# Gram products of two chunks on four corners of the array instead of two

## What is computed

```python
k_n = k / (np.linalg.norm(k, axis=-1, keepdims=True) + 1e-06)
state = np.zeros((B, H, D, D))
for t in range(S):
    kt, vt, bt = (k_n[:, :, t], v[:, :, t], beta[:, :, t, None])
    y[:, :, t] = einsum('bhd,bhde->bhe', q[:, :, t], state)
    v_old = einsum('bhde,bhd->bhe', state, kt)
    state = state + bt[:, :, :, None] * einsum('bhd,bhe->bhde', kt, vt - v_old)
x = y as (B * S, H * D)
# experts: out[mask] = gate_w * eom * (relu(x[mask] @ w1[e]) @ w2[e]), e = argmax(x @ w_gate)
# last layer: maximum(x @ w1, x @ w2, x @ w3) @ w_out
```

## Time and profile before

| | us |
|---|---|
| median of three runs | 1061.64 |
| the runs | 1056.43 to 1076.32 |
| the profiled execution | 1061.8 |
| its span | 1060.1 |
| attention stage, without its start and end | 60 to 420 |
| TensorE busy over the span | 1008.5 (95%) |
| vector engine busy | 522.3 (49%) |
| ScalarE busy | 375.6 (35%) |
| GpSimd busy | 364.0 (34%) |

### The profile page before, as it was taken

One profiled execution on the slowest core, in us unless ns is written; L12 is line 12 of the kernel. 1 busy time (PEld: TensorE's weight loads), 2 busy tenths in 40 slices (PEclk: granted clock), 3 DMA queues, 4 the chain that ended last, 5 costly groups with the idle time before them and its releaser, 6 DMA issues. The chain is left out here.

```text
span 1060.1 us, 28043 instructions
## 1 busy us (share of the span) xinstructions
PE 1008.5 (95%) x11748; PEld 883.5 (83%) x11748; DVE 522.3 (49%) x1109; ACT 375.6 (35%) x735; POOL 364.0 (34%) x275
## 2 busy tenths in 40 slices
PE   3899999999999999789999999998999999999998
PEld 3788888888888888669999999997788888888987
DVE  5567667775677765354444443442433333323332
ACT  3556566565566666122222222221312121212110
POOL 4545376554535342133564552634301010100000
PEclk9899999998999999689999999999999999999999
DMA  9222222221222120234542445322201010100000
GB/s 302 100 57 60 58 75 66 67 67 50 65 68 67 51 60 17 95 130 172 179 171 92 149 154 171 134 90 82 60 30 34 26 37 22 37 30 8 23 8 30
DMA packets 58044, 84.66 MB, mean 80 GB/s; under 512 B 28880, under 2 KB 52944, under 8 KB 55376
## 3 DMA queue, kind: packets, MB, share of 16 engines
q1 hardware_dynamic: 52272, 46.89, 14.3%
q0 software_dynamic: 5664, 36.18, 9.9%
HBM read 61.62 MB, written 21.43 MB: 78 GB/s over the span
## 5 line engine op out<-in xcount | busy, mean ns | idle before, releaser
L1159 PE MATMUL hb<-early,last_h 128*128 128x512 f32 x648 | 206.0, 399 | 0.5 <-DVE early L1303 0.5
L1159 PEld LDWEIGHTS hb<-early,last_h 128*128 128x128 f32 x648 | 120.4, 189 | 28.3 <-DVE early L1303 0.9
L1159 PE MATMUL hb<-early,last_l 128*128 128x512 f32 x324 | 128.4, 396 | 0.0
L750 POOL TENSOR_TENSOR n_base<-n_kb_a,cf 128x512 f16<-128x512 f32 x24 | 30.4, 1268 | 167.8 <-DVE n_kb_a L600 167.8
L610 DVE TENSOR_TENSOR p<-bank,cf 128x512 f16<-128x512 f32 x96 | 66.2, 690 | 36.0 <-PE bank L379 34.9
L552 ACT CAST t<-bank 128x512 f16<-128x512 f32 x96 | 56.5, 588 | 66.4 <-PE bank L372 66.1
L1196 POOL DMA_INDIRECT rows<-y_sorted,idx x24 | 24.5, 1022 | 155.1 <-PE ob L1227 151.8
L1159 PE MATMUL ob<-wo_h,early 128*128 128x384 f32 x288 | 75.1, 339 | 0.0
L1083 POOL TENSOR_TENSOR late<-w_raw,late 128x3072 fp32r<-128x3072 f32 x8 | 54.5, 6811 | 59.8 <-DVE late L1023 59.5
L1159 PEld LDWEIGHTS hb<-early,last_l 128*128 128x128 f32 x324 | 61.0, 188 | 14.8
L992 ACT CAST ht_h<-ht_bank 128x512 fp32r<-128x512 f32 x56 | 32.9, 587 | 109.4 <-PE ht_bank L943 55.4
(11 more groups left out here) (173 smaller groups left out, 2205.4 us busy)
## 6 DMA issues: line engine op xcount, KB each, us to landing
w_raw<-w POOLq DMA_DIRECT2D x14, 1536.0 KB, 7.7
kq_t<-qh SPq DMA_DIRECT2D x24, 256.0 KB
y_sorted<-y_sb SPq DMA_DIRECT2D x31, 192.0 KB, 1.9
x_in<-x_sorted SPq DMA_DIRECT2D x29, 192.0 KB, 2.5
k_raw<-kt_in SPq DMA_DIRECT2D x24, 192.0 KB, 2.4
v_in<-vh SPq DMA_DIRECT2D x24, 192.0 KB
k_own<-kh SPq DMA_DIRECT2D x24, 192.0 KB, 2.4
out<-o_sb SPq DMA_DIRECT2D x24, 192.0 KB, 1.8
```

The lines of the kernel that those rows point to most:

```text
L1159: ins = pe.matmul(out, a[x], b[y], start=first and i == 0, stop=last and i == 2, skip_group_check=True)
```

## The change

In `gram` the loops over e and p are exchanged, and the second chunk's head half hh writes to the other partition half, `half[hh ^ e]`. The matmuls of a pair now go to the corners (0, 0), (1, 1), (0, 1) and (1, 0) in turn. Both signals are given in the last turn. For chunk 1 everything that follows has its two heads in swapped partition halves: the keys, values and beta on the host (`crossed`), beta_k, the views from which rhs is formed, and z. As the zeros of z lie in other places for chunk 1, z gets one buffer per chunk.

```diff
+    def crossed(x, heads, chunks):
+        second = np.flip(x, heads)
+        return np.where(np.arange(2).reshape([2 if i == chunks else 1 for i in range(x.ndim)]) == 1, second, x)
+
+    kh = crossed(k.transpose(g, s, st, hh, t, e, p, d), 3, 5).reshape(TILES, P, U, D)
+    vh = crossed(v.transpose(g, s, st, hh, t, e, p, d), 3, 5).reshape(TILES, P, 2, NP, D)
+    bh = np.stack([crossed(beta.transpose(hh, t, g, s, st, e, p), 0, 5).reshape(P, TILES, U),
...
-    z = single("z", [P, NP, 2, D], F32)
+    z = double("z", [P, NP, 2, D], F32)
...
-                for e, out in ((0, ttb), (1, pb)):
-                    for p in range(NP):
-                        for s, r in zip(half, rows):
-                            ins = pe.matmul(out[s, P * p:P * p + P], kq[r, NP * e + p, 0, :], kq[r, NP * e + p, :, :],
+                for p in range(NP):
+                    for e, out in ((0, ttb), (1, pb)):
+                        for hh, r in enumerate(rows):
+                            ins = pe.matmul(out[half[hh ^ e], P * p:P * p + P], kq[r, NP * e + p, 0, :], kq[r, NP * e + p, :, :],
                                             start=p == 0, stop=True, skip_group_check=True)
-                    ins.then_inc(gram_done[st], 1)
+                        if p == NP - 1:
+                            ins.then_inc(gram_done[st], 1)
...
-                                    z[st][:, p].rearrange("q h d -> q (h d)"), start=False, stop=True, skip_group_check=True)
+                                    z[e][st][:, p].rearrange("q h d -> q (h d)"), start=False, stop=True, skip_group_check=True)
...
-                    act.copy(z[st][half[hh], :, hh, :], by_head[0:C, hh]).then_inc(z_out[st], 1)
+                    act.copy(z[e][st][half[hh], :, hh ^ e, :], by_head[0:C, hh]).then_inc(z_out[st], 1)
...
-                    dve.tensor_tensor(rhs[st][s, :, hh, :], v_in[par][st][s, e], by_head[0:C, hh], ALU.subtract).then_inc(rhs_out[st], 1)
+                    dve.tensor_tensor(rhs[st][s, :, hh, :], v_in[par][st][s, e], by_head[0:C, hh ^ e], ALU.subtract).then_inc(rhs_out[st], 1)
...
-                        ins = dve.tensor_tensor(to[half[hh], e], own[half[e], hh], b[half[e], hh], ALU.mult)
+                        ins = dve.tensor_tensor(to[half[hh ^ e], e], own[half[e], hh], b[half[e], hh], ALU.mult)
...
-            dve.memset(z[st][:], 0.0)
+            for e in range(2):
+                dve.memset(z[e][st][:], 0.0)
```

More of the change, by code:

```diff
@@ L94, in layouts @@
     kt = k.transpose(g, s, st, e, t, p, hh, d).reshape(TILES, P, U, D)
-    kh = k.transpose(g, s, st, hh, t, e, p, d).reshape(TILES, P, U, D)
     qh = np.pad(q.reshape(shape).transpose(g, s, st, hh, e, p, t, d), pad).transpose(0, 1, 2, 3, 7, 4, 5, 6)
-    vh = v.transpose(g, s, st, hh, t, e, p, d).reshape(TILES, P, 2, NP, D)
-    bh = np.stack([beta.transpose(hh, t, g, s, st, e, p).reshape(P, TILES, U),
+    def crossed(x, heads, chunks):
[4 more added lines that the diff above has]
+    bh = np.stack([crossed(beta.transpose(hh, t, g, s, st, e, p), 0, 5).reshape(P, TILES, U),
                    beta.transpose(e, t, g, s, st, p, hh).reshape(P, TILES, U)], axis=1)
```

## The result

The changed kernel is slower: 1072.07 us median (1067.63 to 1083.19) against 1064.6 us (1055.07 to 1078.06) for the kernel before on the same chip. The ratio is **1.0105**, 95% interval [1.0076, 1.0134]. It is a ratio of means of runs in the fast state, which leaves out the five slowest of the 20 runs of before (1073.23 us and more); over all runs it would be 1.007. The loss is about 1%, and its interval is clear of 1. The prediction of 1055.1 us had the wrong sign, and the measured time lies above its range (1050 to 1067.5). The profiled execution of the changed kernel took 1076.57 us, 14.8 more than that of before; the two traces thus show about twice the loss of the medians.

A forecast was written before the change was run, and what follows sets the result against it. TensorE looked like the bound of the attention stage, though each Gram product could gain only until p is ready. 1061.8 - 7.0 (earlier updates) + 0.3 (memsets) = 1055.1 us, range 1050 to 1067.5 us.

The forecast's parts named there:

- Length of the product: Gram product on TensorE: four corners run at once, shortening each product by 0.87 us, to about 1.1 us from 1.96.
- rival A: Gram product: corners don't overlap, it keeps 1.80 us and n_base comes later; 1067 us, chance 0.15.
- What of it is felt: Update behind each Gram product starts 0.33 us (stream 0) or 0.25 us (stream 1) sooner; the rest becomes waiting for p.
- Is it given back behind the product: n_kb_a and n_base behind the Gram product: n_base stays where it is and just fits, so nothing is taken off.
- z, heads, layouts: Copies, subtraction, beta_k and loads cost nothing more; two more z memsets at the start cost 0.3 us once.
- The size of the gain: All Gram products of the attention stage: 12 x 0.33 + 12 x 0.25 = 7.0 us off the total.
- The sum: Whole kernel: 1061.8 less 7.0 plus 0.3 gives 1055.1 us.
- Rival B: TensorE's clock: the new pauses of about 0.6 us bring two more falls at 3.3 us each; 1062 us, chance 0.10.
- signs of being wrong: Gram span not halving, update sooner than p + 0.15 us, or more clock stretches at 0.50 between 60 and 420 us.
- Rival C: Gram products: all of the shortening comes through, 20.9 us less; 1041 us, chance 0.05.

The follow-up runs named there:

- z_double: Kernel before with only z doubled (one buffer per chunk) and its two additional memsets, nothing crossed: 1064.43 us, ratio 1.0008.
- after_align: Changed kernel plus 6 small matmuls (8 columns) behind each Gram product from step 3 on, making a step six code packets: 1046.83 us, ratio 0.9933.
- before_align: Kernel before plus the same 6 small matmuls behind each Gram product from step 3 on: 1056.15 us, ratio 0.9975.
- after: The changed kernel as it stands, against the kernel before: 1072.07 us, ratio 1.0105; profiled execution 1076.57 us.
- corners_only: Kernel before with only chunk 1's Gram product written to the two other corners, behind chunk 0; layouts and z left: 1070.35 us, ratio 1.0121.
- after_shift64: Changed kernel plus 64 small matmuls (128 instructions) on TensorE at the idle start: 1068.98 us, ratio 1.0055 to the kernel before.
- fill2: Changed kernel plus two pairs of idle matmuls (512 columns) behind each Gram product, in the wait for p: 1056.29 us, ratio 0.9956 to the kernel before.
- after_align_off: after_align plus 64 small matmuls at the idle start: 1104.83 us median of four runs, ratio 1.024 to 1.047 to the kernel before.

## Why the prediction was wrong, point by point

**Length of the product: right.** 1.10 us for 32 records, four corners at once: (1.10 - 0.27) / 31 = 0.027 us from one record to the next, half of the 0.0545 of before. The rule of the Trainium skill cited in rival A (a load overlaps only where the row group differs) would have kept 1.8 us; the measurement decides against it for 64x64 tiles of this form.

**What of it is felt: right.** The update starts 1.47 and 1.55 us behind the product's start, p + 0.15 us, 0.33 and 0.25 us sooner. The rest is the wait for p, though the waits view shows only 7.0 us of it: it counts from the modelled end of the last Gram record (0.37 for 0.58).

**Is it given back behind the product: right as far as it went.** n_kb_a's pieces are back to back (1.28 us); n_base ends 3.87 us behind the product's start, before 4.04, a little sooner than forecast.

**z, heads, layouts: right.** z_double shows no difference in time. The first Gram product starts at 11.53 instead of 11.18 us, 0.35 later; the forecast was 0.3.

**The size of the gain: right at one place of the code.** after_align against before_align: last product 372.2 against 378.8, 6.6 us less, and medians 9.3 us apart; the sum said 7.0 less 0.3. Their eight steps from 3 on differ by 4.9 us (264.6 and 269.5), where 8 x 0.58 = 4.6 were forecast; each trace has one fall of the clock in them. At the other place the same two kernels stand the other way round: last product 425.7 against 405.0. So 7.0 us is not what the shorter product is worth in itself; its worth depends on where the borders of the code fall.

**The sum: here is the step that failed.** It took 7.0 us off and let the rest of the program move up as it stood. It held no term for "issue", although the trace of before had pauses of 0.5 to 1.7 us in TensorE's own issue, one of which I quoted. I took them for a property of the kernel, and priced only a new wait and the clock falls. The pauses hang on how far each code packet starts ahead of its first instruction, and with a product 0.3 us shorter six of them (ahead of records 3179, 5768, 6138, 6507, 7247, 7986) came 42 to 88 matmuls later, at places where in this trace of before they had come in time. Measured between 60 and 420 us: +8.7 us of issue, and up to 11.9 us of clock.

**Rival B had half of it.** It named the clock and gave 1062 us for two more falls. One of the prediction's own signs of being wrong came true here: five stretches at 0.50 between 60 and 420 us instead of two. But it hung the falls on the new 0.6 us waits. The five falls in after all stand behind issue pauses of 1.1 us and more, and after_align, which has the waits for p as well (5.8 us), has one fall in its last eight steps, behind an issue pause of 0.85 us, and a clock of 0.99. **Rival A** came near the measured time (1067) for a reason that was false; the four corners overlap. **Rival C** fell with the wait for p.

**What stays open.** Why a shorter product makes TensorE ask for a packet later. From the product's start to record 6425, where before gets its packet, the order of TensorE's instructions and of the loads in the trace is the same in before and corners_only; only the spacing differs, 0.3 us in the product and 0.15 us in a small pause that both have once a step (0.50 us before, 0.65 in corners_only, at record 6390). Whether the engine's look-ahead, its queue of loads and matmuls or another reader of the code decides it, no run here separates. Nor was a case run in which the same borders are held at a third place, so how wide the good places are is not known. In after and after_shift64 the steps with borders 42 to 65 matmuls behind stream 0's product took 32.5 to 33.0 us from step 3 on; in after_align, with borders at about 55, they took 32.1 to 34.7, and in fill2, with 34 to 58, 33.3 to 36.4.

## What to carry to other kernels

In a kernel that issues some 45 TensorE instructions per us, look at the "issue" rows of TensorE's waits before costing an edit; if they carry more than a few us, a gain of a fraction of a us per step can turn either way, and a small difference in time between two versions may be code placement and not the edit. Test it cheaply: put some tens of tiny instructions where the engine idles at the start, and compare; if the time moves, count the instructions of a step, pad them to a whole number of code packets, and compare the versions again at more than one shift, since here the order of the two kernels turned with it. Change one thing at a time by what the trace shows, not by what the edit is called: "crossed but in series" had the shorter product too.

## What the runs showed of the hardware

TensorE's code arrives while the kernel runs, in packets of 16 KB, 256 instructions (six of them in 739.5 matmuls); where one starts late, the engine stands still for 1 to 2.9 us at the packet's border and goes on 2.2 to 2.9 us behind the packet's start.

Pauses of 1 us and more were often, not always, followed by 3.4 to 13.7 us at 1.2 GHz, which costs up to half of that time: in after_align_off the clock's mean over eight steps is 0.87, in after_align 0.99. In each of the aligned kernels 3.4 us at 1.2 GHz stand behind a pause of 0.85 us.

Two pairs of 64x64 corners overlap fully, f32, 48 rows, 128 columns: 1.10 us for 32 matmuls in rotation, 1.59 in two series of 16 one behind the other, 1.96 on one pair of corners.
